# One recurrent attention and two gated layers on one core: where alpha's range is checked, and how the reciprocals of its running product are made

## What is computed

```python
for t in range(S):                                   # S = 768
    state = alpha[:, :, t, :, None] * state + einsum('bhd,bhe->bhde', k[:, :, t], v[:, :, t])
    y[:, :, t] = einsum('bhd,bhde->bhe', q[:, :, t], state)
x = y.transpose(0, 2, 1, 3).reshape(B * S, H * D)    # 3072 tokens x 384
x = (sigmoid(x @ w_gate) * (x @ w_val)) @ w_out      # layer 1, 1536 wide
h = maximum(maximum(x @ w1, x @ w2), x @ w3)         # layer 2, 768 wide
out = h @ w_out2
```

## Time and profile before

| what | value |
|---|---|
| runs | 896.21, 897.68 and 897.45 us, median 897.45 |
| profiled execution | 895.64 us |
| its span | 893.8 us |
| PE busy | 863.2 us, 97% of the span |
| DVE, ACT, POOL busy | 414.2, 263.0 and 120.5 us |
| chain that ended last | PE 92%, DVE 4%, issue 1%, DMA 1%, ACT 1% |

### The profile page before, as it was taken

One profiled execution on the slowest core, in us unless ns is written; L12 is line 12 of the kernel. 1 busy time (PEld: TensorE's weight loads), 2 busy tenths in 40 slices (PEclk: granted clock), 3 DMA queues, 4 the chain that ended last, 5 costly groups with the idle time before them and its releaser, 6 DMA issues.

```text
span 893.8 us, 13520 instructions
## 1 busy us (share of the span) xinstructions
PE 863.2 (97%) x5213; PEld 802.5 (90%) x5213; DVE 414.2 (46%) x730; ACT 263.0 (29%) x502; POOL 120.5 (13%) x95
## 2 busy tenths in 40 slices
PE   4499999999999999999999999999999999999997
PEld 3489999999999999999999999998888888888886
DVE  7988566366456545545646532232323223232321
ACT  4534333232332232232233233431212212121311
POOL 4355312011011111101101101610000000000000
PEclk9799999999999999999999999999999999999999
DMA  7471021021021021021021020300000000000000
GB/s 296 157 310 45 8 89 45 8 90 45 1 98 45 1 95 45 1 97 45 1 95 45 1 78 5 137 1 1 1 35 1 35 0 35 0 35 0 13 22 35
DMA packets 15602, 46.88 MB, mean 52 GB/s; under 512 B 2112, under 2 KB 6080, under 8 KB 15552
## 3 DMA queue, kind: packets, MB, share of 16 engines
q1 hardware_dynamic: 15552, 46.15, 14.4%
HBM read 40.24 MB, written 4.72 MB: 50 GB/s over the span
## 4 chain that ended last, share of the span: by engine, by line
PE 92%; DVE 4%; issue 1%; DMA 1%; ACT 1%; POOL 0%; SPq 0%; ACTq 0%; DVEq 0%; POOLq 0%
PE ps_out L815 17%; PE ps_gate L790 16%; PE ps_val L790 16%; PE ps_gate L796 8%; PE ps_val L796 8%; PE ps_out L888 6%; PE ps_sc L790 5%; PE ps_sc L796 3%; PE ps_sc L748 3%; PE ps_y L779 2%; PE ps_sc_odd L888 2%; PE ps_y L775 2%; PE ps_y L757 2%; PE ps_y L734 1%; DVE rdec L560 1%
## 5 line engine op out<-in xcount | busy, mean ns | idle before, releaser
L790 PE MATMUL ps_gate<-x_hi,w_hi 128*128 128x384 f32 (+1 forms) x396 | 139.8, 353 | 2.9 <-ACT x_hi L381 2.9
L790 PE MATMUL ps_val<-x_hi,w_hi 128*128 128x384 f32 (+1 forms) x396 | 140.3, 354 | 0.9 <-DVE h_sb L622 0.9
L790 PE MATMUL ps_gate<-x_hi,w_lo 128*128 128x384 f32 (+1 forms) x396 | 139.1, 351 | 0.0
L790 PE MATMUL ps_val<-x_hi,w_lo 128*128 128x384 f32 (+1 forms) x396 | 138.4, 349 | 0.0
L622 DVE TENSOR_TENSOR h_sb<-act_sb,ps_val 128x384 f32<-128x384 f32 x96 | 52.7, 549 | 148.3 <-PE ps_val L796 148.0
L796 PE MATMUL ps_gate<-x_lo,w_hi 128*128 128x384 f32 (+1 forms) x396 | 118.1, 352 | 0.0
L796 PE MATMUL ps_val<-x_lo,w_hi 128*128 128x384 f32 (+1 forms) x396 | 117.0, 349 | 0.0
L381 ACT ACTIVATE h_hi<-h_sb 128x384 fp32r<-128x384 f32 x96 | 50.4, 525 | 159.7 <-DVE h_sb L622 159.6
L422 ACT ACTIVATE act_sb<-ps_gate 128x384 f32<-128x384 f32 x96 | 47.2, 491 | 165.2 <-PE ps_gate L796 164.9
L707 DVE TENSOR_TENSOR probs<-probs,ps_val 128x512 f32<-128x512 f32 x36 | 24.7, 687 | 137.8 <-PE ps_val L796 137.8
L601 DVE TENSOR_TENSOR h_lo<-h_sb,h_hi 128x384 fp32r<-128x384 f32 x96 | 60.5, 630 | 52.0 <-ACT h_hi L381 52.0
(11 more groups left out here) (98 smaller groups left out, 1260.7 us busy)
## 6 DMA issues: line engine op xcount, KB each, us to landing
inbuf<-att_in SPq DMA_DIRECT2D x23, 704.0 KB, 5.6
mid<-w SPq DMA_DIRECT2D x12, 576.0 KB, 9.6
inbuf<-att_in SPq DMA_DIRECT2D x23, 256.0 KB, 2.9
mid<-alpha_flat SPq DMA_DIRECT2D x8, 576.0 KB, 6.3
inbuf<-w SPq DMA_DIRECT2D x6, 768.0 KB, 4.2
out<-inbuf SPq DMA_DIRECT2D x5, 768.0 KB, 3.5
x_raw<-y_last SPq DMA_DIRECT2D x48, 24.0 KB, 1.9
out<-inbuf SPq DMA_DIRECT2D x4, 192.0 KB, 2.1
```

What stands on the lines that cost most here:

```text
L790: mm(bank, w_at(half, f, c + k * P, total=total), x_hi[:, k, 0:w], start=(k == 0 and half == 0), stop=False)
```

## The change

The eight extra pieces of alpha and everything that works on them are gone, and so is the clamp. In their place ACT checks each chunk's own alpha in place, after the reciprocals have been made: an Abs of alpha minus 1, then a Relu of that minus 0.25 whose sum goes into a column of `viol` (two activations of 128x512, 24 times). SP may load the next chunk over a buffer only when its check is done too (`viol_done`). The columns are summed on DVE at f = 1 of the last tile of layer 1, transposed on PE at f = 3 and made into the flag at f = 5. The four engines read the flag at the very end of their programs (SP before its store loop, branching behind it) and with the flag set would run the general attention and then `slow_layers`, a second copy of both layers, which was not there before. `x_final` is gone; ACT waits for the six small transfers directly.

The four reciprocals of 112x128 become one reciprocal of the four last columns (112x4) and four scans of 112x127 that run backward from it, each step multiplying by alpha: rdec at t is rdec at t+1 times alpha at t+1.

In the opening the constants are loaded after chunk 1 rather than before it, weight pieces 0 to 5 are loaded with no other traffic between, all three pieces' `split_w1` on POOL come after the chunks, and DVE and ACT run in another order.

```diff
 SP
+                    sp.wait_ge(viol_done, 5 - Cs)
+            def load_w1(f):
+                if f >= RING:
+                    sp.wait_ge(w_hi_done, f - RING + 1)
+                    sp.wait_ge(w_lo_done, f - RING + 1)
+                elif f >= RING - 2:
+                    sp.wait_ge(y_done, 3)
+                    sp.wait_ge(viol_done, 3)
+                sp.dma_start(slot(f), w1[f]).then_inc(stage_in[f % RING], 16)
...
             load_chunk(0, 0)
+            load_chunk(1, 0)
             sp.dma_start(cst[:, :], consts).then_inc(consts_in, 16)
-            load_chunk(1, 0)
...
+            load_w1(0)
             load_chunk(2, 0)
+            for f in range(1, RING - 2):
+                load_w1(f)
+            load_chunk(4, 0)
+            load_chunk(3, 0)
             move_last(0)
+            for f in range(RING - 2, NF1):
+                load_w1(f)
...
             sp.wait_ge(stored, 16 * (TILES2 - 1 + SUB))
+            with sp.If(bad):
+                general()
+                slow_layers()
 ACT
-                            act.wait_ge(x_final, T + 2)
+                            act.wait_ge(last_moved[0], 32 * T + 64)
...
+                    if att_next and f in (2, 5, 8):
+                        check(CPT * (Ts + 1) + (f - 2) // 3, i)
...
+            def check(Cs, i):
+                C = Cs + 6 * i
+                act.wait_ge(rdec_done, C * PAIRS + PAIRS)
+                a = buf_cols(buf(Cs), 0, PAIRS * CH)
+                nc.scalar.activation(a, a, ACT.Abs, bias=minus_one).then_inc(dist_done, 1)
+                act.wait_ge(dist_done, C + 1)
+                col = viol[:, bass.ds(C, 1)]
+                nc.scalar.activation(a, a, ACT.Relu, bias=minus_range, accum_out=col).then_inc(viol_done, 1)
...
+                    if f == 0:
+                        check(2, 0)
+                    split_w1(f + 3)
 DVE
-                nc.vector.tensor_scalar(att(buf(Cs), ALPHA), att(buf(Cs), ALPHA), 1 - ALPHA_RANGE, 1 + ALPHA_RANGE,
-                                        ALU.max, ALU.min).then_inc(clamp_done, 1)
...
+                    nc.vector.reciprocal(rdec[0:PR, par, :, CH - 1], decay[0:PR, par, :, CH - 1]).then_inc(rend_done, 1)
+                    nc.vector.tensor_copy(d_end[0:PR, par, :], decay[0:PR, par, :, CH - 1]).then_inc(end_done, 1)
...
-                    nc.vector.reciprocal(rdec[0:PR, Cs % 2, p, :], decay[0:PR, Cs % 2, p, :]).then_inc(rdec_done, 1)
...
+                    nc.vector.tensor_tensor_scan(rdec[0:PR, par, p, CH - 2::-1], att(buf(Cs), ALPHA)[:, p, CH - 1:0:-1],
+                                                 zero[0:PR, :].broadcast_to([PR, CH - 1]), rdec[0:PR, par, p, CH - 1:CH],
+                                                 ALU.mult, ALU.add).then_inc(rdec_done, 1)
...
+            layer1(TILES - 1, 0, False, {1: sum_violations, 5: set_flag})
 PE
-            pe.wait_ge(flag_step, 1)
-            nc.tensor.transpose(ps_gate[0:1, 0:P], amax[:, NA:NA + 1], ident).then_inc(flag_t, 1)
-            pe.wait_ge(flag_ready, 1)
-            bad = pe.value_load(flag_i[0:1, 0:1], min_val=0, max_val=1)
...
+            layer1(TILES - 1, 0, False, True, {3: flag_row})
```

More of the change, by code:

```diff
@@ L187, in build, with staged @@
         HALVES = (slice(0, D), slice(ODD, PR))
-        ring = ([("w", 0), ("a", 0), ("a", 1), ("a", 2), ("w", 1), ("a", 3), ("chunk", 2), ("chunk", 2)]
-                + [("a", n) for n in range(4, NA)] + [("w", n) for n in range(2, NF1)])
-        place = {item: n for n, item in enumerate(ring)}
-        def staged(eng, item):
-            n = place[item]
-            loads = sum(m % RING == n % RING and ring[m][0] != "chunk" for m in range(n + 1))
-            eng.wait_ge(stage_in[n % RING], 16 * loads)
+        def staged(eng, f):
+            eng.wait_ge(stage_in[f % RING], 16 * (f // RING + 1))
         block = ctx.enter_context(nc.Block())
@@ L358, in _ @@
             scale_qk(1, 0)
-            split_w1(0)
             scale_qk(2, 0)
-            for f in range(1, NF1):
+            for f in range(NF1):
                 split_w1(f)
@@ L470, in _ @@
             khs_copy(2, 0)
-            distance(5)
-            distance(6)
+            split_w1(2)
             y_copy(2, 0)
-            for n in range(7, NA):
-                distance(n)
-            split_w1(2)
             for k in range(KT):
@@ L844, in layer1, with flag_row @@
                         out1(Ts - 1, i, NF1 - 1)
+                    if f in hooks:
+                        hooks[f]()
+            def flag_row():
+                pe.wait_ge(flag_step, 1)
+                nc.tensor.transpose(ps_sc_odd[0:1, 0:P], viol[:, CHUNKS:CHUNKS + 1], ident).then_inc(flag_t, 1)
             def general():
```

381 lines of the change are left out of this document (236 added, 145 removed).

## The result

The changed kernel takes 901.25 us (median of 7 runs, 900.21 to 905.08) beside 897.41 for the kernel before on the same chip: 1.005 of it, 95% interval 1.0037 to 1.0064. It is slower by 3.8 us. 890.5 was forecast, with a range to 894.3, and faster with a chance of 0.92.

A forecast was written before the change was run, and what follows sets the result against it. PE was taken as the bound, with the gain in when layer 1 starts: -7.1 (gate product) - 0.9 + 0.7 (first steps) + 0.4 (end) = -6.9 us, median 890.5, range 887.0 to 894.3.

The forecast's parts named there:

- What bounds the kernel: PE, busy 97% of the span; beyond 90 us freeing other engines gains at most 1.1 us, so the opening decides.
- rival D: Gain eaten elsewhere: late constants, weight piece or chunk behind viol_done, or a full fetch at the end; 895.7 us, chance 0.08.
- First scores and chunk 0: Opening: scores start at 8.5 us, not 10.19, released by the constants; attention of chunk 0 ends at 16.5, against 18.49.
- Chunk 1: Opening: scores 1.9 us, transposes 0.6, outer product 1.2, attention 2.15, ending at 23.3; the check costs 0.35 on the path.
- the clock: Opening: PE's clock may fall to 1.2 GHz inside the chain, 0 to 3.5 us more; 0.8 taken, y out at 32.4.
- Chunk 2: Opening: khs waits behind ACT's weight piece, 0.8 us of new wait; last copy of y ends at 31.6, against 38.15.
- The join and the first steps: Layer 1's start: gate product ends at 39.35, shift 7.1 us; then -0.9 for earlier state, +0.7 for val at low clock.
- The end: Span's end: SP's branch behind its last wait costs 0 to 1.8 us, 0.4 taken; other engines finish before the last transfer.
- A: DVE's scans lock with POOL and run slower backward; only 2.5 to 5 us gained, about 893.6, chance 0.20.
- B: Opening chain runs at the high clock throughout; 9 to 10.5 us gained, about 887.8, chance 0.11.
- C: Check becomes ACT's bound in layer 1's steps, from 2.81 us a check; at 3.3 us +4.6, 902.0, chance 0.03.
- three signs of a wrong forecast: PE's first product after 38; waits beyond 90 us over 2 us; over 1.5 us from last transfer's landing to span's end.

The follow-up runs named there:

- e1: Kernel before, with SP no longer waiting for the y_last transfers, so chunk loads go out early: 903.94 us beside 897.95, ratio 1.007.
- e10: Changed kernel with only PE's loop over tiles 1 to 6 written out, loads still early: 888.72 us, ratio 0.9904.
- e14: Kernel before with only PE's loop over tiles 1 to 6 written out: 894.89 us, ratio 0.9975.
- e11: Changed kernel with SP waiting for the six y_last transfers before the next chunk loads, SP's loop written out: 902.15 us, ratio 1.0062.
- e15: Changed kernel with chunk loads held until PE is past the back edge and 148 unused semaphore increments on PE ahead of layer 1: 917.65 us.
- e9: Changed kernel, next tile's first chunk loaded early, second held past PE's back edge, SP's branch ahead of the final wait for stores: 894.46 us.
- e13: e10 plus constants loaded first, khs of chunk 2 ahead of the weight piece, SP's and ACT's branches hidden: 889.95 us, ratio 0.9917.
- e16: e13 without PE's flag load, its branch and its part of the general path: 887.79 us, ratio 0.9896.
- e8: Changed kernel with the backward scans replaced by reciprocals as in the kernel before: 904.8 us, ratio 1.0091.
- e12: Changed kernel without the two check activations per chunk and SP's waits for them: 901.04 us, ratio 1.0048.
- e6: Changed kernel with 20 unused semaphore increments on PE ahead of layer 1, loop head at instruction 1022: 899.0 us, ratio 1.0017.

## Why the prediction was wrong

**What bounds the kernel, and rows 2.** Here is the step that failed. It said that from 90 us to the end PE waits 1.1 us, so that an edit which only frees another engine there "is worth at most that". That bounds a gain, not a loss. Those 1.1 us stood at the two back edges and were the wait for PE's code, read as one for `x_hi`; the fetch was served just in time. In the trace of before the packet of code travels at 252.0 and the loads' traffic starts at 252.5. I priced each wait that SP gained (`viol_done`) and none that it lost (`moved`, the branch, `x_final`). The sum had no term for loads that start earlier, and rival D looked only for loads that come later. Measured: +5.7 and +6.1 in the profiled execution. Nor had it a term for the place of the loop's head, which the change moved by 20 instructions. e1 shows the part of the loads by itself (6.0), and e10 that the back edges are the error: 888.72 against the 890.5 forecast. That this is so close is partly luck. Writing the loop out also takes away 2.4 that the kernel before has (e14), and the opening and the end were mis-sized the other way. Against e14 the change is worth 6.2, where the sum said 6.9. The page of before reads 4 in its first two slices, not only in the first: PE's share is low up to 44.7 us, which changes nothing in the sum.

**First scores and chunk 0.** Right: 8.46 against 8.5, released by the constants; attention 14.48 to 16.4 against 14.5 to 16.5.

**Chunk 1 and the clock.** The prices at the high level were used too early: transposes 1.01 and not 0.6, outer product 1.81 and not 1.2, attention until 25.6 and not 23.3. The sum's 0.8 for the clock should have been about 3.5 in this execution, where y is out at 35.1 against 31.6 without that term, and 2.5 in the mean of eleven. In the executions with the same opening code y was out between 31.2 (e11, outer product of chunk 1 at 1.03) and 35.4 (e15, 1.81), 34.1 in the mean of eleven, against 32.4 forecast. At the second milestone (before: 105.8) ten of them have 96.0 to 101.6, mean 99.5, so the profiled 101.29 is one of the slower openings. A shift of 6.3 to the forecast 7.3.

**Chunk 2.** The wait for `khs` behind the weight piece was forecast (0.8) and is there, with 1.78. A check costs 0.71 + 0.73 + 0.19 us on ACT (1.6 with the gaps, 1.25 forecast): the third item is a read of the accumulator that no row of before had. ACT's groups over the whole span:

```profile
L498 ACT ACTIVATE inbuf<-inbuf,cst 128x512 f32<-128x512 f32 x23 | 16.7, 725 | 2.2
L495 ACT ACTIVATE inbuf<-inbuf,cst 128x512 f32<-128x512 f32 x23 | 16.3, 708 | 0.0
...
L498 ACT ACTIVATION_READ_ACCUMULATOR inbuf<-inbuf,cst x18 | 3.4, 186 | 0.0
```

**The join and the first steps.** Right in kind: the first product waits for `x_hi`, 4.88 us, with the flag out of its way, and the 0.89 before val of step 1 is gone. The val product at the low level took 2.9 and not 1.5, so the term was +1.4 and not +0.7.

**The end.** Mis-sized: 2.0 and not 0.4. The 0.4 for SP's branch is about right: e9, which hides it, gains 0.4. The other 1.6 is the last store, which lands later because a packet of PE's code travels amid it (e13, e16). I had argued that PE would "finish earlier than the last transfer". It does, but its code is still fetched then, and I left out that this can hold up the transfer. The sign that I had named for it, more than 1.5 us between the last landing and the span's end, did not show it: that is 0.8.

The Trainium skill (Runtime: NRT & Kernel Launch, Instruction fetch mechanics) was cited for the end, at 1.4 more. The trace has 1.6 more, by the way just told. The same section says that any taken branch whose target is not among the fetched pages forces a fetch by DMA, and that this is one reason why kernels prefer to be unrolled. I applied it to the branch that the change adds and not to the two that were there all along: e10 and e14 bear it out, with 12.5 and 2.4 us.

**Rivals.** A: the backward scans are dearer than forward ones, 637 ns against 462 in the mean over the span, and 474 against 400 in the median; e8 shows that they still pay. B did not come: chunk 1 of this execution ran at the low level. C: the check does not bound the kernel (e12: 0.2 us). D had the direction of the error, a gain eaten elsewhere, and not its mechanism or size. Of the three signs of a wrong forecast two came: PE's first product started at 38.35, after 38, and the waits beyond 90 us were 9.6 and not under 2.

## What to carry to other kernels

When an edit lets a queue run ahead, ask what else uses the DMA engines at that time: not only data, but the code that an engine fetches at the back edge of a long loop. Look for back edges of the bounding engine in the timeline before a change, and write that loop out if it is taken few times; here that one line is worth more than the whole change. A small wait in the trace bounds what can be gained at a place and says nothing about what can be lost there. And check the name that a profile gives to a wait against the time at which the named engine was done.

## What was not expected of the hardware

- PE's wait at a back edge ranges from 0.4 to 4.9 us, by the traffic at that time and by where the loop's head stands in PE's code: 20 to 30 instructions more, which do nothing, shortened it by 1 to 2.3 us. With no loads in flight the first of the two packets of code starts 2.0 to 3.5 us ahead of the edge with the head at 1002, 6.0 at 1022 and 6.7 at 1032. The Trainium skill (Runtime: NRT & Kernel Launch, Instruction fetch mechanics) says that code comes in blocks of 256 instructions, and 1002 lies 22 short of such a boundary. That the boundary is what matters is not shown: the head at 1022 (e6) is short of it too and has the two packets apart as at 1032.
- A packet of code of 16 KB takes 0.9 to 2.2 us at the edges, and PE's first product follows 1.6 to 2.4 us after its end.
- After the waits of 2.9 us and more the granted clock was at the level of 1.2 GHz for the gate product or most of it and often into the val product, at a cost of 1.3 to 2.7 us. After waits of up to 1.3 us it stayed at 2.4 GHz.
- A packet of code amid a store made its last part land 1.5 us later (e13 against e16).
- An increment of a semaphore takes PE 150 ns (e15).
- The opening of the same code took 31.2 to 35.4 us until y was out, by when the clock rose from 1.2 to 2.4 GHz.
